# Strassen first layer: the sums of the first two blocks move from PSUM to SBUF, and with them the second input of their maxima

## What is computed

```python
x = attention(q, k, v, mem_k, mem_v)           # 3072 x 512
h = np.maximum(np.maximum(x @ w1, x @ w2), x @ w3)   # 512 -> 768
x = h @ w_out                                  # 768 -> 512
h = x @ w_in                                   # 512 -> 2048, then a clipped square, then @ w_out2
```

## Time and profile before

| | |
|---|---|
| median of three runs | 962.69 us (962.04 to 963.97) |
| the profiled execution, whole launch | 960.89 us |
| its span, first to last instruction | 959.1 us |
| granted TensorE clock, mean | 0.999 |
| TensorE busy | 942.9 us (98%) |
| VectorE busy | 485.6 us |
| ScalarE busy | 435.4 us |
| GpSimd busy | 457.1 us |

### The profile page before, as it was taken

How to read it: one execution, slowest core, us unless ns; L and a number is a source line. 1 busy time by engine, 2 the same in 40 slices (tenths; PEclk the granted TensorE clock), 3 DMA queues, 4 the chain that set the end, 5 groups by cost and what they waited for, 6 DMA issues and landing times.

```text
span 959.1 us, 19061 instructions
## 1 busy us (share of the span) xinstructions
PE 942.9 (98%) x7806; PEld 876.4 (91%) x7806; DVE 485.6 (51%) x755; ACT 435.4 (45%) x713; POOL 457.1 (48%) x628
## 2 busy tenths in 40 slices
PE   5999999999999999999999999999999999999998
PEld 5999999899999999999989899898999898989897
DVE  4673566677756795761344432545334453423232
ACT  3342343433333443433545555645556463645354
POOL 1669997868976593130232423333332323232321
PEclk9999999999999999999999999999999999999999
DMA  9777899999799878882536445445464443545321
GB/s 371 262 280 254 308 333 396 393 412 386 238 383 368 268 266 306 277 310 102 183 120 226 154 176 187 176 153 185 153 233 143 154 162 137 197 179 182 121 99 66
DMA packets 50328, 223.01 MB, mean 233 GB/s; under 512 B 5953, under 2 KB 10049, under 8 KB 42689
## 3 DMA queue, kind: packets, MB, share of 16 engines
q0 software_dynamic: 31936, 165.17, 48.1%
q1 hardware_dynamic: 18304, 56.63, 16.4%
HBM read 178.00 MB, written 43.78 MB: 231 GB/s over the span
## 4 chain that ended last, share of the span: by engine, by line
PE 96%; DVE 2%; DMA 1%; issue 1%; ACT 0%; SPq 0%; DVEq 0%; ACTq 0%
PE mlp_ps L647 22%; PE mlp_ps L648 21%; PE mlp_ps L649 21%; PE attn_ps L649 4%; PE attn_ps L648 4%; PE attn_ps L647 3%; PE scores_ps L649 3%; PE scores_ps L648 3%; PE scores_ps L647 3%; PE attn_ps L640 3%; PE scores_ps L611 2%; PE trans_ps L649 2%; PE trans_ps L648 2%; PE trans_ps L647 2%; PE trans_ps L620 1%; DMA qk_raw<-qk_l 1%
## 5 line engine op out<-in xcount | busy, mean ns | idle before, releaser
L936 ACT ACTIVATE up_m<-mlp_ps 128x384 f32<-128x384 f32 x292 | 142.4, 489 | 301.9 <-PE mlp_ps L649 278.3
L647 PE MATMUL mlp_ps<-yc,wa 128*128 128x384 f32 x472 | 160.0, 339 | 1.9 <-ACT up_m L936 1.8
L648 PE MATMUL mlp_ps<-yc,wa 128*128 128x384 f32 x472 | 158.3, 335 | 0.0
L649 PE MATMUL mlp_ps<-yc,wa 128*128 128x384 f32 x472 | 157.9, 335 | 0.0
L544 POOL CAST wo<-wo_raw 128x1024 fp32r<-128x1024 f32 x32 | 33.3, 1040 | 193.5 <-PE trans_ps L649 187.3
L523 POOL DMA_DIRECT2D wa<-wa_scratch x59 | 31.7, 538 | 193.0 <-PE mlp_ps L649 192.0
L647 PE MATMUL mlp_ps<-yc,wb 128*128 128x384 f32 x354 | 119.2, 337 | 0.0
L648 PE MATMUL mlp_ps<-yc,wb 128*128 128x384 f32 x354 | 118.8, 336 | 0.0
L649 PE MATMUL mlp_ps<-yc,wb 128*128 128x384 f32 x354 | 118.3, 334 | 0.0
L1537 DVE SCALAR_TENSOR_TENSOR ramp<-ramp,up_m 128x768 f32<-128x768 f32 x62 | 59.4, 958 | 109.1 <-ACT ramp L1185 109.1
L647 PEld LDWEIGHTS mlp_ps<-yc,wa 128*128 128x128 f32 x472 | 88.6, 188 | 9.2 <-ACT up_m L936 3.6
(11 more groups left out here) (178 smaller groups left out, 2179.0 us busy)
## 6 DMA issues: line engine op xcount, KB each, us to landing
wa<-wa_scratch POOLq DMA_DIRECT2D x59, 1024.0 KB, 5.4
wb<-wb_scratch POOLq DMA_DIRECT2D x59, 768.0 KB, 6.7
qk_raw<-qk_l SPq DMA_DIRECT2D x24, 768.0 KB, 9.1
wo_raw<-w_out POOLq DMA_DIRECT2D x32, 512.0 KB, 4.0
wa_scratch<-stage_a POOLq DMA_DIRECT2D x30, 512.0 KB, 5.0
v_raw<-v_l SPq DMA_DIRECT2D x24, 512.0 KB, 7.1
wb_scratch<-stage_a POOLq DMA_DIRECT2D x30, 384.0 KB, 6.6
y_raw<-y_scratch SPq DMA_DIRECT2D x8, 768.0 KB, 5.0
```

Of the source, the lines that this page charges most:

```text
L647: pe.matmul(out_ap, a_hi, b_hi, start=first, stop=False, skip_group_check=beside)
L648: pe.matmul(out_ap, a_lo, b_hi, start=False, stop=False, skip_group_check=beside)
L649: return pe.matmul(out_ap, a_hi, b_lo, start=False, stop=last, skip_group_check=beside)
L936: return act.activation(o, i, ACT.Copy)
```

## The change

All four sums now go to SBUF: to `h_run` for m = 0, and to `snap` for m = 1 and 2. Every maximum then reads both of its inputs from SBUF, and TensorE waits for the sum alone (`summed`) before it begins a bank, in all places where it waited for the maximum. `bank_read` is gone. The number of instructions is the same on every engine.

```diff
-            def bank_read(g, b):
-                if g % 3 and b < 2:
-                    pe.wait_ge(merged, merges(g) + b + 1)
-                else:
-                    pe.wait_ge(summed, 4 * g + b + 1)
 # l1_product
                 elif q and i < 3:
-                    bank_read(g - 1, (0, 1, 3)[i])
+                    pe.wait_ge(summed, 4 * (g - 1) + (1, 2, 4)[i])
 # l2_blocks
                     elif x < 2:
-                        bank_read(last_pair, x)
+                        pe.wait_ge(summed, 4 * last_pair + 1 + x)
 # product
                 if g == 0 and i < 2:
-                    bank_read(PERIODS_S - 1, i)
+                    pe.wait_ge(summed, 4 * (PERIODS_S - 1) + 1 + i)
 # block_sum
-                if m == 0:
-                    to = h_run[:, f, t]
-                else:
-                    to = l1_bank(g, i) if b < 2 else snap[:, f, t]
-                dve.tensor_tensor(to, snap[:, f, t], l1_bank(g, i), ALU.add).then_inc(summed, 1)
+                to = snap if m else h_run
+                dve.tensor_tensor(to[:, f, t], snap[:, f, t], l1_bank(g, i), ALU.add).then_inc(summed, 1)
 # block_max
-                new = l1_bank(g, (3, 5)[b]) if b < 2 else snap[:, f, t]
-                dve.tensor_tensor(h_run[:, f, t], h_run[:, f, t], new, ALU.max).then_inc(merged, 1)
+                dve.tensor_tensor(h_run[:, f, t], h_run[:, f, t], snap[:, f, t], ALU.max).then_inc(merged, 1)
```

## The result

The changed kernel has a median of 970.62 us (969.97 to 971.43, six runs); the kernel before, on the same chip, 962.46 us (961.53 to 963.97, six runs). The ratio is 1.0086, 95% interval 1.0076 to 1.0096: slower by 8.2 us. The forecast was 963.6 us with a range up to 965.3. The profiled execution took 970.5 us, its span is 968.7 us, and the granted clock is 1.00 (of 2.4 GHz) throughout.

What follows compares the result with a forecast made beforehand. The prediction took TensorE, busy for 98% of the span, as the bound. Stall growth of 0.74 + 0.24 less 0.03 us for shorter instructions gave +0.95 us: 962.69 to 963.64 us, range 962.0 to 965.3.

Steps and rivals of the forecast that it cites:

- Maximum 0 at 163.61 keeps GpSimd out until 164.01: First tile, q = 1: maximum 0 goes through undelayed and GpSimd's line 504 starts 0.24 us later than its 163.77.
- the two stalls: TensorE's waits for ScalarE's copy near 170 and 278 us, pair q = 1 of tiles one and two: 0.39 and 0.69 us.
- other 32: Remaining new maxima: mostly only GpSimd blocked, 0.1 to 0.2 us; the worst 0.8 us late, covered by 1.95 us VectorE idle.
- The rule of the Trainium skill: VectorE with two SBUF inputs and GpSimd reading SBUF: second to start fully blocked; stalls would grow 1.28 us, not 0.98.
- Maximum 1: Near 165.6 and 273.5 us: waits for line 506's end plus 0.41 us, about 1.1 us long, 0.54 us later in tile one.
- stall 1: First tile, q = 1, TensorE's wait for ScalarE's copy near 170 us: grows by 0.74 us.
- stall 2: Second tile, q = 1, TensorE's wait for ScalarE's copy near 278 us: grows by only 0.24 us.
- The relief: TensorE's earlier release from its wait for a maximum: taken as 0; as a rival 0 to −0.4 us, 0.20 including no effect.
- The sums: Sums written to SBUF instead of PSUM: median 547 instead of 561 ns, 14 ns less each.
- The third tile: Its twelve new maxima meet almost no GpSimd work (17.91 of 69.30 us); none of them becomes long.
- Rival (b): First tile's loads of `wa` and `wb`: GpSimd runs late, TensorE waits for weights; 965.2, up to 967.6 us; chance 0.10.
- Rival (c): Both stalls at their bounds, 2.0 us, or one covered maximum laid bare, 1.75 us: 964.6 us; chance 0.10.

Runs made afterwards that it cites:

- b0_psum: Changed kernel with block 0's sum and maximum back in PSUM form, TensorE waiting for that maximum: 961.78 us against 961.49 before, ratio 1.0002.
- small_sub: Changed kernel with GpSimd's lines 504 and 506 cut to 8 columns in the Strassen pairs: 962.86 us, ratio 1.0011 to the kernel before.
- before_small_sub: Kernel before with GpSimd's lines 504 and 506 cut to 8 columns in the Strassen pairs: 962.85 us, ratio 1.0014 to the kernel before.
- pool_waits: Changed kernel with one more wait, so GpSimd starts line 504 only when maximum 0 is done: 963.22 us, ratio 1.0012 to the kernel before.
- gap_506: Changed kernel with GpSimd waiting for its own line 504 ahead of line 506: 967.04 us against 961.5 before, one execution.
- micro: Separate kernel without attention or matmul: VectorE's sum and maximum against two GpSimd subtractions at shifted starts, 126 scenes; only its rows count, not its time.
- micro2: Second such kernel without attention or matmul, 112 scenes, varying the first GpSimd operation and what precedes it; only its rows count, not its time.
- load_after_504: Changed kernel with GpSimd's load of wa moved from ahead of line 504 to between lines 504 and 506: 962.38 us, one execution.
- b1_psum: Changed kernel with block 1 put back to PSUM, block 0 staying in SBUF: 975.52 us, ratio 1.0149 to the kernel before.
- late_release: Changed kernel with TensorE waiting for the maxima of blocks 0 and 1 again before their banks: 973.22 us, ratio 1.0116 to the kernel before.

## Why the prediction was wrong, point by point

**The step that failed** is "Maximum 0 at 163.61 keeps GpSimd out until 164.01, so line 504 starts 0.24 us later", and with it "nothing is blocked but GpSimd" for the remaining pairs. It compared the maximum's start with that of line 504 alone and took for granted that the maximum goes through. The row of after at 164.07 shows the opposite: 2.88 us for the maximum, 1.31 us for line 504. What stood directly ahead of line 504 is in the trace of before, just ahead of the earlier trace rows, and has no place in the forecast:

```profile
163.20 0.56 POOL L523 DMA_DIRECT2D wa<-wa_scratch  x1 [1.69 <-PE mlp_ps L649]
```

It starts 0.41 us ahead of the maximum at 163.61. Two of the eight long maxima stand in the pairs of the two stalls, where the forecast gave maximum 0 no delay at all; the other six are among the "other 32". For each, a term of 2.3 to 2.4 us on VectorE was missing.

The evidence for the step was thin: one case, line 484 held by 0.22 us, an operation of 128 columns with no DMA issue directly ahead. It was carried over to a 512-column operation behind a DMA issue, and that is the very case in which the runs show the long wait. The forecast's form of the blocking (wait to the end, then 0.41 us) was right: with the end of line 506 it gives all eight long maxima of after to 0.02 us. What it lacked was that GpSimd's stretch begins with the DMA issue, and that behind one two operations without a gap can count as one.

**The rule of the Trainium skill** (SBUF — State Buffer, Who interferes with whom), by which issue order decides and the second is fully blocked, was read in the prediction as a reason to hold GpSimd a little longer. Without a DMA issue ahead the runs agree with its order: out of idle a subtraction that starts 0.02 us first makes the maximum wait, and at 0.00 us the maximum wins. Behind an issue they agree only if the issue counts as GpSimd's start; by the start of the subtraction they don't, since the maximum that started 0.19 us ahead of it was the one blocked. And the block does not end with the first operation: it lasts to the end of the second subtraction, 2.88 to 2.97 us in after. The measurement decides.

**Maximum 1 and the two stalls.** Right in kind, too large: in b0_psum 0.87 us instead of 1.1, stall 1 up by 0.20 instead of 0.74, and stall 2 down by 0.30 instead of up by 0.24. Where the whole change is in, maximum 1 at 167.46 takes 0.56 us, because maximum 0 has pushed it behind line 506, and the waits for ScalarE's copies stay at 1.7 us.

**The relief, taken as 0, with 0.4 us as the other end.** Nothing in the runs is against it: small_sub and before_small_sub differ by 0.01 us, and such a pair can tell about 1 us. **The sums:** 549 ns against 547, right. **The third tile:** free of all this, right, 72.7 against 72.8 us.

**The rivals.** None had the mechanism. Rival (b) named late weights, and those cost 0.3 us in after. Rival (c) came nearest in place (late maxima) but stopped at 2.0 us, because each term was bounded by one operation of GpSimd. The sentence under "other 32 maxima", that 0.8 us would go to TensorE if the cover of 1.95 us idle time were gone, was the right thought with the wrong size: a maximum that is 2.4 us late goes through any such cover.

**How far it is settled.** Shown by runs: block 0's maximum carries the whole loss (b0_psum); what makes it long is that it starts while GpSimd is in a stretch of DMA issue, line 504 and line 506 without a gap (pool_waits and gap_506, which open a gap ahead of line 504 and behind it; micro and micro2, which leave out the issue); nothing else in the change counts by more than about 1 us (small_sub against before_small_sub). Open: why behind a DMA issue the waiting maximum is not let in between the two subtractions, why 128 columns or a cast let it in at the end of the issue, and why the maximum at 196.31 us in before was not held. The runs show that it is so and no more.

No version tried beats the kernel before. b0_psum, half of the change, equals it (1.0002); the nearest with all of the change in it are pool_waits (+0.12%) and load_after_504 (962.38 us, one execution), and both only take the loss back.

## What to carry to other kernels

Before VectorE's second input is moved from PSUM to SBUF, look at what GpSimd does at that time, its DMA issues included. Where an issue stands directly ahead of its operations, count its stretch from the issue, and price the instruction up to the end of the last operation that follows without a gap, not of one. Then ask who is queued behind it on VectorE: here it was not the maximum that TensorE missed but the sum and the softmax step behind it. A blocking rule read from one short example is worth as much as that example; if the pattern at stake (here DMA issue, long operation, next operation, all without a gap) is not in the trace, its bound is the whole pattern.

## What the runs showed of the hardware that was not expected

- A VectorE instruction with two SBUF inputs that starts up to 0.28 us (micro kernels: 0.48 us) ahead of a two-input GpSimd operation can still have to wait for that operation and the next, 2.9 us instead of 0.56, if GpSimd's DMA issue directly ahead of them started at least 0.11 us before it (0.32 to 0.39 us in after). Where it started ahead of the issue it took 0.56 us (three times in after).
- Without the DMA issue, a waiting VectorE instruction gets in at the boundary of two gapless GpSimd operations, and the second of them is held. The trace of the kernel before has such a place outside the change; VectorE, then GpSimd:

```profile
101.36 1.66 DVE L1317 TENSOR_TENSOR h_lo<-h_max,h_hi 128x384 fp32r<-128x384 f32 x1
```

```profile
100.86 0.51 POOL L494 CAST stage_a<-stage_a 128x384 fp32r<-128x384 f32 x1
101.33 1.28 POOL L504 TENSOR_TENSOR stage_a<-w_raw,stage_a 128x512 fp32r<-128x512 f32 x1
102.56 1.33 POOL L506 TENSOR_TENSOR stage_a<-stage_a 128x384 fp32r<-128x384 f32 x1
```

  Lines 504 and 506 again, without a gap, but behind a cast: the VectorE instruction ends 0.41 us after line 504, and line 506 takes 1.33 instead of 1.02 us.
- Held by a GpSimd operation, a maximum of 384 columns ends 0.41 to 0.43 us after that operation's end; one that wins holds GpSimd for 0.2 to 0.4 us.
- Behind stalls of TensorE the granted clock fell in some executions: in b1_psum to 0.87 between 197 and 201 us, where TensorE was busy for 1.71 us, and to 0.71 between 201 and 205 us (a cost of at most 1.7 us by the estimate above), in late_release to 0.57 between 313 and 317 us. In after it stayed at 1.00 in every stretch shown.
